# The last step of feed-forward 1 with its sums in two row halves of TensorE's array

## The reference

```python
def _attn_ref(r, k, v, w, u):                 # B=4, H=8, S=768, D=48
    state = zeros((B, H, D, D)); y = zeros_like(r)
    for t in range(S):
        cur = einsum('bhd,bhe->bhde', u[None] * kt, vt)
        y[:, :, t] = einsum('bhd,bhde->bhe', rt, state + cur)
        state = wt[:, :, :, None] * state + einsum('bhd,bhe->bhde', kt, vt)
    return y

def _moe_ref(x, w_in, w_out):                 # feed-forward 1
    h = x @ w_in
    return (h * clip(h + 3.0, 0.0, 6.0) / 6.0) @ w_out

def _moe2_ref(x, w_in, w_out):                # feed-forward 2
    h = x @ w_in
    return (h * (1.0 / (1.0 + exp(-h)))) @ w_out
```

## Time and profile before

| | |
|---|---|
| time, median of 3 runs | 977.9 us |
| the three runs | 974.6, 977.9, 979.27 us |
| profiled execution, first to last instruction (span) | 976.2 us |
| its mean granted TensorE clock | 0.981 |
| busy: TensorE, its weight loads | 949.0 us (97%), 827.5 us (85%) |
| busy: VectorE, ScalarE, GpSimd | 489.5 (50%), 306.9 (31%), 142.8 us (15%) |
| mean of a matmul record, L633 to L635 | 391 to 393 ns |
| sums1 in all (6 steps) | 288 matmuls on each of three lines |

### The profile page before, as it was taken

How to read it: one execution, slowest core, us unless ns; L and a number is a source line. 1 busy time by engine, 2 the same in 40 slices (tenths; PEclk the granted TensorE clock), 3 DMA queues, 4 the chain that set the end, 5 groups by cost and what they waited for, 6 DMA issues and landing times.

```text
span 976.2 us, 13697 instructions
## 1 busy us (share of the span) xinstructions
PE 949.0 (97%) x5084; PEld 827.5 (85%) x5084; DVE 489.5 (50%) x723; ACT 306.9 (31%) x493; POOL 142.8 (15%) x134
## 2 busy tenths in 40 slices
PE   6779999999999999999999999999999999999998
PEld 6768887888888788888888889999999999999997
DVE  7866746663765566376634553333233332333332
ACT  2232223223222322222234453233233332332322
POOL 5733302320422133023200000000000000000000
PEclk7779999999999999999999999999999999999999
DMA  8551130303110211303020200000000000000000
GB/s 230 187 166 54 53 105 1 105 0 105 52 52 25 80 52 52 104 1 105 0 97 33 98 33 1 1 32 0 0 32 0 32 0 0 32 0 0 33 1 33
DMA packets 13366, 48.52 MB, mean 50 GB/s; under 512 B 1568, under 2 KB 2208, under 8 KB 13344
## 3 DMA queue, kind: packets, MB, share of 16 engines
q1 hardware_dynamic: 13344, 48.23, 15.8%
HBM read 43.50 MB, written 4.72 MB: 49 GB/s over the span
## 4 chain that ended last, share of the span: by engine, by line
PE 89%; DVE 3%; issue 2%; POOL 2%; DMA 2%; ACT 1%; SPq 0%; DVEq 0%; ACTq 0%; POOLq 0%
PE bank L621 14%; PE bank L623 13%; PE bank L622 13%; PE bank L645 7%; PE bank L647 7%; PE bank L646 7%; PE bank L633 6%; PE bank L635 6%; PE bank L634 6%; PE bank L696 4%; PE bank L677 2%; PE bank L693 2%; PE bank L687 2%; DMA x<-w_fm 1%; DVE tmp L492 1%
## 5 line engine op out<-in xcount | busy, mean ns | idle before, releaser
L621 PE MATMUL bank<-x_hi,w_hi 128*128 (+1 forms) x576 | 231.9, 403 | 1.2 <-DVE x_lo L533 1.2
L623 PE MATMUL bank<-x_hi,w_lo 128*128 (+1 forms) x576 | 227.8, 395 | 0.0
L622 PE MATMUL bank<-x_lo,w_hi 128*128 (+1 forms) x576 | 227.2, 394 | 0.0
L356 ACT CAST g_hi<-g 128x512 fp32r<-128x512 f32 x192 | 119.1, 620 | 289.0 <-PE bank L647 144.3
L464 DVE TENSOR_TENSOR g<-g,bank 128x512 f32<-128x512 f32 x96 | 65.9, 687 | 244.4 <-ACT g L350 244.4
L471 DVE TENSOR_TENSOR g_lo<-g,g_hi 128x512 fp32r<-128x512 f32 x192 | 145.0, 755 | 0.9 <-ACT g_hi L356 0.9
L348 ACT ACTIVATE g<-bank,half 128x512 f32<-128x512 f32 x96 | 66.2, 689 | 215.8 <-PE bank L623 215.0
L466 DVE SCALAR_TENSOR_TENSOR g<-g,bank 128x512 f32<-128x512 f32 x96 | 65.9, 687 | 132.6 <-ACT g L348 132.6
L647 PE MATMUL bank<-w_hi,g_lo 128*128 128x384 f32 x384 | 129.5, 337 | 0.0
L645 PE MATMUL bank<-w_hi,g_hi 128*128 128x384 f32 x384 | 129.5, 337 | 0.0
L623 PEld LDWEIGHTS bank<-x_hi,w_lo 128*128 128x128 f32 x576 | 108.8, 189 | 24.1
(11 more groups left out here) (82 smaller groups left out, 873.5 us busy)
## 6 DMA issues: line engine op xcount, KB each, us to landing
unit_in<-rkv_tm SPq DMA_DIRECT2D x23, 576.0 KB, 6.4
unit_in<-rk_fm SPq DMA_DIRECT2D x23, 448.0 KB, 4.2
x<-w SPq DMA_DIRECT2D x8, 768.0 KB, 4.8
unit_in<-w SPq DMA_DIRECT2D x8, 768.0 KB, 4.3
unit_in<-w_fm SPq DMA_DIRECT2D x23, 226.2 KB, 2.9
out<-tmp SPq DMA_DIRECT2D x5, 768.0 KB, 3.3
out<-tmp SPq DMA_DIRECT2D x4, 192.0 KB, 1.9
x<-rkv_tm SPq DMA_DIRECT2D x1, 576.0 KB, 14.8
```

Source lines behind the costliest of these rows:

```text
L356: nc.scalar.copy(g_hi[:, p, :], g[:, p, :]).then_inc(ghi_done, 1)
L621: nc.tensor.matmul(h_ps[j % 2][:, :], wh, xh, start=k == 0, stop=False)
L622: nc.tensor.matmul(h_ps[j % 2][:, :], wh, xl, start=False, stop=False)
L623: last = nc.tensor.matmul(h_ps[j % 2][:, :], wl, xh, start=False, stop=k == KT - 1)
```

## The change

In the last step of feed-forward 1, and only there, `sums1` is replaced by `sums1_halves`. Each of the nine matmuls of a tile is done as two, one that contracts rows 0 to 63 and one that contracts rows 64 to 127, issued in turn, each with its own weight load. The upper halves add up in acc[0] to acc[2] as before, the lower halves in att[0] to att[2]. After the copies of `sums_out`, VectorE adds the three banks of att to x2 in three additions that count in a new semaphore, halves_added. ScalarE's `x2_hi` waits for it, and TensorE waits for it before the first sums of feed-forward 2. The wait stands in the loop of feed-forward 2, so that it is passed five times; its value doesn't change.

```diff
@@ scalar: x2_hi
                 act.wait_ge(sums_a, 2 * c + 3)
                 act.wait_ge(sums_v, c + 2)
+                if some(c):
+                    act.wait_ge(halves_added, KT)
                 for k in range(KT):
@@ vector: end of the last step
             sums_out(c)
+            dve.wait_ge(sums_a, 2 * c + 3)
+            dve.wait_ge(sums_v, c + 2)
+            for m in range(KT):
+                nc.vector.tensor_tensor(x2_step(c, m), x2_step(c, m), att[m][:, :], ALU.add).then_inc(halves_added, 1)
             wlo(CHUNKS + 7)
@@ tensor
+            def sums1_halves(n, j):
+                pe.wait_ge(glo_done, n + 1)
+                if j % 4 == 0:
+                    pe.wait_ge(*split(2 * (j // 4) + 1))
+                for m in range(KT):
+                    wh, wl = w_out(w_hi, j, m, P), w_out(w_lo, j, m, P)
+                    gh, gl = g_hi[:, j % 2, :], g_lo[:, j % 2, :]
+                    for x, (wt, gt) in enumerate([(wh, gh), (wh, gl), (wl, gh)]):
+                        for top, out_bank in ((0, acc[m]), (ODD, att[m])):
+                            last = nc.tensor.matmul(out_bank[:, :], wt[top:top + ODD], gt[top:top + ODD], start=j == 0 and x == 0,
+                                                    stop=j == FT - 1 and x == 2)
+                last.then_inc(summed, 1)
@@ tensor: last step, both of its loops
-                sums1(FT * c + j - 2, j - 2)
+                sums1_halves(FT * c + j - 2, j - 2)
@@ tensor: loop of feed-forward 2, j == 2
                         pe.wait_ge(sums_a, 2 * (STEPS + c) + 1)
                         pe.wait_ge(sums_v, STEPS + 2 * c + 1)
+                        pe.wait_ge(halves_added, KT)
                     sums2(FT * (STEPS + c) + j - 2, j - 2)
```

More of the change, by code:

```diff
@@ L137, in build @@
         x2hi_done = sem("x2hi_done")
+        halves_added = sem("halves_added")
         g_done = sem("g_done")
```

## The result

The change makes the kernel slower: 983.98 us (median of 5 runs, 981.6 to 988.71) against 977.97 us (median of 5, 974.6 to 981.68). The ratio is 1.0079, with a 95% interval of 1.0049 to 1.0109. The profiled execution spans 982.3 us against 976.2.

A forecast was written before the change was run, and what follows sets the result against it. The prediction took TensorE's matmul stream, bound by columns, as the bound. Pairs 0, switches 5.1 and additions 1.9 us summed to 7.0, added to a median of 977.9 for 984.9 us, range 978 to 998.

The forecast's parts named there:

- The pairs: Sums blocks of feed-forward 1's last step: 144 half-height pairs overlap wholly, 0.227 us each like one full-height matmul, costing 0.
- rival prices (0.30, 0.38, 0.45 a pair): Sums pairs: partial overlap (0.30, chance 0.09), or none, with loads (0.38) or matmuls (0.45) one after the other (chance 0.12).
- The switches: Between hidden and half-height sums: each change of height costs 0.19 us, 27 of 32 count, 5.1 us.
- Four switches hidden by the stall for g_lo: Where TensorE idles for g_lo, between 565.6 and 572.8: four switches, 0.76 us, vanish in that stretch.
- The additions: Before feed-forward 2's first sums: TensorE waits for three VectorE additions, so sums2 starts 1.87 us late.
- g_lo of tile 1 and the last w_lo chunk stay covered: VectorE behind the additions: both come 0.54 us later, but TensorE needs that g_lo 1.87 later, so nothing is lost.
- The whole: Whole kernel: 7.0 us more than the runs' median of 977.9, giving 984.9 us, 0.7% slower.
- The first rival: Edges of sums blocks: switches below 0.11 us each, only the additions' 1.9 us left, 979.8 us; chance 0.14.

The follow-up runs named there:

- 64 more switches: Three pairs per block halved, each followed by two full-height matmuls, against the same pairs issued together: stretch 102.37 us against 88.86.
- 14 fewer: The change with order hidden, hidden, sums, sums in the first 14 blocks, against the same order at full height: stretch 85.74 us against 80.78.
- the last block alone: Only the last of the 16 blocks in halves, additions and waits as in the change, against the kernel before: stretch 82.56 us against 80.80.
- nine uppers first: The change with each block's nine upper-row matmuls issued before its nine lower-row ones, against the change: stretch 109.35 us against 88.93.
- three and three: The change with three upper-row, then three lower-row matmuls, three times in a block, against the change: stretch 89.05 us against 88.93.

## Why the prediction was right

- **The pairs: 0 forecast.** Right. All rival prices (0.30, 0.38, 0.45 a pair) are out, and the step from fp32 scores with 128 columns to fp32r sums with 512 held. In the change two pairs start 0.232 us apart on the mean, and the prediction had named any pitch other than 0.227 as a sign of being wrong. But the 0.005 more are not the pairs': single full-height matmuls behind the stall of the kernel before start 0.234 apart too (573.18 to 574.82 in the earlier trace rows, seven distances), and pairs far from a switch 0.228.
- **The switches: 0.19 each, 5.1 us forecast.** The mechanism was right, the size too small. All that the stretch lost besides the additions is 8.13 - 1.77 = 6.4 us. The two late starts cost 0.20 on the way in and 0.21 on the way out. The seven distances behind them are 0.232 (pairs) and 0.230 (hidden) in place of 0.227, which adds 0.035 and 0.023, so a switch costs 0.235 us where a whole block follows: 27 x 0.235 = 6.3. With 64 more switches it came to 0.211, because there only two or three matmuls stand between two of them, and with 14 fewer to 0.23. For the same reason a block of hidden and halves takes 4.55 us (513.39 to 517.94), 0.47 more than 4.08 where 0.38 was forecast. Why the distances stay long for a while, no run shows; the hidden blocks of feed-forward 2 have them too, behind sums of 384 columns and with no idle time before (0.231 on the mean in the kernel before). The way in is made of the two parts that were read from the scores: 0.09 before the first start, then 0.11 before the second, the load in the open. The second part is no matter of height: the stall at 572.84 has the same 0.34 to the second start. By the rule in the Trainium skill, "TensorEngine Tiling (Array Packing)", section Key Properties, the change of height drains TensorE, and the traces agree wherever the height changes; the drain alone would have been less than half of it.
- **Four switches hidden by the stall for g_lo.** Right: the edge at 576.82 shows 0.06 us above a plain switch, where the prediction had left about 0.2. The difference is the size of the four switches again.
- **The additions: 1.87 us forecast.** Measured 1.77 (4.09 - 2.32) in the change and 1.76 with the last block alone. The three take 1.88 us, against 1.89 for L566's three. The 0.1 too much lies behind them: sums2 starts 0.11 after the last addition ends (583.14 to 583.25), where the sum had 0.06 for the signal and 0.11 for a load. A load in the open shows in both kernels alike (the second matmul of sums2 follows the first by 0.25 in place of 0.17, 577.14 to 577.39 before and 583.25 to 583.49 after), so it is no part of the difference. That g_lo of tile 1 and the last w_lo chunk stay covered held: no time is lost behind the stretch.
- **The whole.** 7.0 us forecast. The stretch lost 8.1, the profiled spans differ by 6.1, the medians by 6.0, and the ratio's interval, 4.8 to 10.7 us of 977.97, holds all of these. That the spans and the medians come within 1 us of the forecast is partly luck: the profiled execution of after came to the stretch 2.0 us sooner, and whole times scatter by more than that. By the stretch the forecast was 1.1 too small. The first rival, switches too cheap to be told, had put the limit at 0.11 us each; they cost about twice that.

## What to carry to other kernels

Half-height matmuls of different rows run side by side and cost one full-height matmul for each pair, so halving a contraction that already fills 128 rows gained nothing here; it added 0.21 to 0.24 us for every change between full and half height, plus the extra banks to be added up. Where half-height work is there anyway (two contractions of 64), keep it in one run and count the changes of height, not the matmuls. And where a consumer waits for several evacuations, wait for the one whose bank it takes: that was worth 1.2 us here with one number.

## What the runs showed of the hardware

TensorE starts matmuls out of their program order when they lie on other rows: in the kernel with nine uppers first, the first lower one started 0.01 us after the sixth upper, with three uppers before it in the program not yet started, and with three and three every pair overlapped (89.05 us against 88.93 in turn). In no run did one pass more than three, although nine stood before it in the first of these kernels; what sets this was not tried. The Trainium skill, "TensorE: Matmul & The Clock Gate", section The mechanism, says that matmuls keep the order of the program in start and end; between row halves the starts in these two traces disagree. Of the ends nothing can be said, since they are modelled in the profile.

The Trainium skill, "TensorE: Matmul & The Clock Gate", section Measured speedup vs the span model, gives 3.07x for four row tiles of 512 columns, and the prediction had estimated from it a pair a third longer than a single matmul. That loss was not met with two row halves: they reach 2 x 0.227 / 0.232 = 1.96 in the blocks of the change, and 2 x 0.227 / 0.228 = 1.99 far from a switch. Four row tiles were not run here.
